# Attention, two feed-forward stages on one core: order of the outputs, of the first step, and products of zeros at the start

## The chip, the cores and the metric

The kernel runs on 1 core of one Trainium2 chip. The metric is the device time of one execution, in microseconds (us), as the median over several runs. A profile is one execution taken by the hardware profiler; its own time and its span (first to last instruction) are given beside it.

## The reference

Inputs are q, k, v of 8 batches x 8 heads x 576 positions x 64, and the weights of two feed-forward stages. What is computed, cut to its core:

```python
gamma = 1.0 - 2.0 ** (-5.0 - np.arange(H))
Dmat = np.where(rel >= 0, gamma ** rel, 0.0)           # rel = query position - key position
attn = ((q @ k.T) / sqrt(64) * Dmat) @ v               # per batch and head, no softmax
x = attn.transpose(0, 2, 1, 3).reshape(4608, 512)
h = max(max(x @ w1, x @ w2), x @ w3);  x = h @ w_out   # 512 -> 768 -> 512
a = x @ u1;  b = x @ u2;  out = ((a * b) @ u3) @ uo    # 512 -> 1024 -> 1024 -> 512
```

All arrays are fp32.

## The kernel before

The first part, up to about 184 us, is the attention. Heads are taken in pairs (32 pairs n, 64 + 64 rows of a 128-partition tile), two pairs a step, 17 steps m. Positions are cut into 4 chunks of 128 and a tail of 64. Inside a chunk the scores are computed and decayed directly; across chunks a 64x64 state per head and chunk is carried. For a pair:

- `scores(n)` (TensorE, L929, L934): products of k and q of each chunk into PSUM.
- `decay_scores(n)`, `decay_tail(n)` (VectorE, L770, L778): scores times a table of decays, into `probs`.
- `decay_values(n)` (ScalarE, L633): v times a table, into `vdec`, in two instructions a pair.
- `sum_state(n)` (TensorE, L949): products of k and `vdec` per chunk, into PSUM bank 6 (`S_STATE`).
- `make_state(n)` (VectorE, L791, L794): the running state of each chunk from these sums, 8 instructions.
- `decay_queries(n)` (GpSimd, L551): q times a table.
- `query_state(n)` (TensorE, L965): decayed queries times the state, 128x128 by 128 columns, into the output's PSUM bank.
- `values(n)` (TensorE, L976): `probs` times v, added there.
- `read_values(n)` (ScalarE, L642): the output of the pair from PSUM into `xst`, one of two buffers; it waits for the stores of pair n - 2.
- `store_x(n)` (SP, L381): two transfers of each pair's output to DRAM.

Step m takes scores, decay and state sums of pairs 2m and 2m + 1 (`made_in`), and queries, values and outputs of pairs 2m - 2 and 2m - 1 (`read_in`). From step 3 on TensorE also computes the product of u3 and uo (`wc_quarter`, L991 to L995, into bank 7, `S_WC`), so that the last two products of the reference become one. All orders are written out by hand, engine by engine, and semaphores join them; an engine takes its instructions in order. On TensorE a step is scores of both pairs, parts of the weight product, queries, state sums, values. `scores(n)` waits from pair 2 on for decays of the step before, and from pair 4 on for `x_out`, the output copies of pair n - 4. On ScalarE a step is splits of weights, `decay_values` of the next step's pairs, `read_values` of this step's.

All transfers are issued by SP, in one queue. Ahead of the steps SP issues q and k, tables, v and the k of the first pairs; in step m it issues loads of weights, k of pairs 2m + 2 and 2m + 3 (each waits for a state sum that frees its buffer), q and k of pairs 2m + 4 and 2m + 5, and then v, store, v, store: v of pairs 2m + 4 and 2m + 5, outputs of 2m - 2 and 2m - 1.

The second part, stages B, C, I and O, multiplies the tokens by the weights, each product as three products of split operands (L1026 to L1028). The change doesn't touch it.

Of the kernel before, what the change touches and what calls it, by code (L numbers as in the profile page):

```python
# [4 lines left out]
P = 128  # L5
BATCH, HEADS, SEQ, DH = 8, 8, 576, 64
# [8 lines left out]
CH = 128  # L15
NC = SEQ // CH
# [149 lines left out]
def made_in(m):  # L166
    return [n for n in (2 * m, 2 * m + 1) if n < NP]


def read_in(m):  # L170
    return [n for n in (2 * m - 2, 2 * m - 1) if n >= 0]


def quarters(m):
    if m >= STEPS - 2:
        return range(QUARTERS - 4 * (STEPS - m), QUARTERS - 4 * (STEPS - m) + 4)
    return range(2 * (m - WC_FROM), 2 * (m - WC_FROM) + 2) if m >= WC_FROM else ()
# [18 lines left out]
def build(nc, qk, vv, kk, wB, wC, wI, u3T, uo, decay, qdecay, vdecay, outT):  # L196
    f32, f32r = mybir.dt.float32, mybir.dt.float32r
# [10 lines left out]
    with ctx:  # L208
# [40 lines left out]
        o = H_AT + 4 * N * 4  # L249
# [5 lines left out]
        o = 50176  # L255
# [25 lines left out]
        o += 2 * NC * CH * 4  # L281
        state = [at(f"state{i}", [P, NC, P], f32, o + i * NC * P * 4) for i in range(2)]
        o += 2 * NC * P * 4
        assert o <= 150528

        ps = ctx.enter_context(nc.psum_tensor("ps", [P, 8, 512], f32))
# [2 lines left out]
        S_STATE, S_WC = 6, 7  # L289

        def sem(name):
            return ctx.enter_context(nc.semaphore(name))

        zeroed = sem("zeroed")
        qk_loaded = [sem(f"qk_loaded{i}") for i in range(4)]
        v_loaded = [sem(f"v_loaded{i}") for i in range(6)]
# [326 lines left out]
        def _(act):  # L623
# [14 lines left out]
            def read_values(n):  # L638
                act.wait_ge(valued, n + 1)
                if n >= 2:  # L640
                    act.wait_ge(x_stored[n % 2], 32 * (n // 2))
                nc.scalar.copy(xst[:, n % 2, :],  # L642
                               ps[:, 2 * (n % 2):2 * (n % 2) + 2, :].rearrange("p a b -> p (a b)")[:, 0:SEQ]
                               ).then_inc(x_out, 1)
# [11 lines left out]
            def read_wc(kb):  # L656
                act.wait_ge(wc_done, kb + 1)
                if kb:
                    act.wait_ge(wc_stored, 32 * kb)
                nc.scalar.copy(wcst[:, :, :].rearrange("p n c -> p (n c)"), ps[:, S_WC, :]).then_inc(wc_out, 1)  # L660
# [9 lines left out]
            def split_tokens(tau, pos):  # L670
# [11 lines left out]
                    act.wait_ge(prod, DONE[(last_of(tau - 1), USED_BY[pos])])  # L682
                nc.scalar.copy(chi[st][pos][:, :, :], raw_block(tau, pos)[:, :, :]).then_inc(c_hi, 1)  # L683

            for n in made_in(0):
                decay_values(n)
            for m in range(STEPS):
                if m in U3_SPLIT:
                    split_u3(U3_SPLIT[m])
                for i in UO_SPLIT.get(m, ()):  # L690
                    split_uo(i)
                if m in WC_READ:
                    read_wc(WC_READ[m])
                for n in made_in(m + 1):
                    decay_values(n)
                for n in read_in(m):
                    read_values(n)
                if m in P1_W_HI:
                    split_weight(P1_W_HI[m], 0)
                    split_weight(P1_W_HI[m], 1)  # L700
                if m in P1_HI:
                    split_tokens(0, P1_HI[m])
# [55 lines left out]
        def _(dve):  # L758
# [3 lines left out]
            def decay_scores(n):  # L762
                p = n % PAIRS
                dve.wait_ge(scored, n + 1)
                if n < 3:
                    dve.wait_ge(dec_loaded[n], 16)
                if n >= 4:
                    dve.wait_ge(valued, n - 3)
                for h in range(2):
                    nc.vector.tensor_tensor(  # L770
                        probs[n % 4][:, h, 0:NC * CH].rearrange("p (n c) -> p n c", c=CH),
                        ps[:, 2 * (n % 2) + h, :].rearrange("p (n c) -> p n c", c=CH),
                        dec[:, 2 * p + h, :].unsqueeze(1).broadcast_to([P, NC, CH]), ALU.mult).then_inc(decayed, 1)
# [8 lines left out]

            def make_state(n):
                p = n % PAIRS
                dve.wait_ge(state_summed, n + 2 - n % 2)
                for c in range(NC):
                    for h in range(2):
                        own = slice(h * DH, h * DH + DH)
                        new = ps[own, S_STATE, (n % 2 * NC + c) * DH:(n % 2 * NC + c + 1) * DH]
                        if c == 0:  # L790
                            nc.vector.tensor_copy(state[n % 2][own, c, own], new).then_inc(state_made, 1)  # L791
                        else:
                            dve.wait_ge(state_made, 2 * NC * n + 2 * (c - 1) + h + 1)
                            nc.vector.scalar_tensor_tensor(  # L794
                                state[n % 2][own, c, own], state[n % 2][own, c - 1, own], CHUNK_DECAY[2 * p + h], new,
                                ALU.mult, ALU.add).then_inc(state_made, 1)
# [17 lines left out]
            def split_tokens(tau, pos):  # L814
                st = tau // TILES
                dve.wait_ge(c_hi, 7 * tau + pos + 1)
                low(clo[st][pos][:, :, :], raw_block(tau, pos)[:, :, :], chi[st][pos][:, :, :]).then_inc(c_lo, 1)

            for i in range(4):
                nc.vector.memset(probs[i][0:TAIL, :, NC * CH:SEQ], 0.0).then_inc(zeroed, 1)  # L820
            for i in range(2):
# [2 lines left out]
            for m in range(STEPS):  # L824
                for n in made_in(m):
                    decay_scores(n)
                for n in made_in(m):
                    decay_tail(n)
                if m in U3_SPLIT:
                    split_u3(U3_SPLIT[m])  # L830
                for i in UO_SPLIT.get(m, ()):
                    split_uo(i)
                if m in P1_W_LO:
                    split_weight(*P1_W_LO[m])
                if m in P1_LO:
                    split_tokens(0, P1_LO[m])
                for n in made_in(m):
                    make_state(n)

            merge = {B: ALU.max, I: ALU.mult}  # L840

# [76 lines left out]
        def _(pe):  # L918
            def scores(n):
                pe.wait_ge(qk_loaded[n % 4], 16 * (n // 4 + 1))  # L920
                if n >= 2:
                    pe.wait_ge(decayed, 3 * (n - n % 2))
                if n >= 4:
                    pe.wait_ge(x_out, n - 3)
                for c in range(NC):
                    for h in range(2):
                        own = slice(h * DH, h * DH + DH)
                        keys = SEQ + c * CH
                        nc.tensor.matmul(ps[:, 2 * (n % 2) + h, c * CH:(c + 1) * CH], qks[n % 4][own, keys:keys + CH],  # L929
                                         qks[n % 4][own, c * CH:(c + 1) * CH],  # L930
                                         start=(c == 0), stop=(c == NC - 1), skip_group_check=True)
                for h in range(2):
                    own = slice(h * DH, h * DH + DH)
                    last = nc.tensor.matmul(ps[:, S_TAIL[h], (n % 2) * TAIL:(n % 2 + 1) * TAIL],  # L934
                                            qks[n % 4][own, KQ_COLS - CH:KQ_COLS], qks[n % 4][own, SEQ - TAIL:SEQ],
                                            start=True, stop=True, skip_group_check=True)
                last.then_inc(scored, 1)

            def sum_state(n):
                pe.wait_ge(v_decayed, 2 * n + 2)  # L940
                pe.wait_ge(k_loaded[n % 2], 16 * (n // 2 + 1))
                if n >= 2:
                    pe.wait_ge(state_made, 2 * NC * (n - n % 2))
                for c in range(NC):
                    for h in range(2):
                        own = slice(h * DH, h * DH + DH)
                        keys = c * P + h * DH
                        at_ = (n % 2 * NC + c) * DH
                        last = nc.tensor.matmul(ps[own, S_STATE, at_:at_ + DH],  # L949
                                                ks[n % 2][:, keys:keys + DH], vdec[n % 2][:, c, own],  # L950
                                                start=(c == 0), stop=(c == NC - 1), skip_group_check=True)
                last.then_inc(state_summed, 1)
# [28 lines left out]
            def wc_quarter(i):  # L981
# [15 lines left out]
                if part == 3:  # L997
                    last.then_inc(wc_done, 1)

            pe.wait_ge(zeroed, 6)  # L1000
            for m in range(STEPS):
                for n in made_in(m):
                    scores(n)
                for i in quarters(m):
                    wc_quarter(i)
                for n in read_in(m):
                    query_state(n)
                for n in made_in(m):
                    sum_state(n)
                for n in read_in(m):  # L1010
                    values(n)
# [102 lines left out]
```

## Time and profile before

| | |
|---|---|
| median of 3 runs | 1265.27 us (1263.46 to 1265.35) |
| profiled execution, its own time | 1261.15 us |
| its span | 1259.4 us |
| granted TensorE clock, mean | 0.997 |
| PE busy | 1223.0 us (97%), 8288 matmuls |
| DVE busy | 787.4 us (63%) |
| ACT busy | 486.6 us (39%) |
| POOL busy | 407.2 us (32%) |

PE is TensorE, DVE is VectorE, ACT is ScalarE, POOL is GpSimd, SP is SyncE, whose queue of transfers is SPq. Busy times are shares of the whole span; the attention part and the four stages after it have limits of their own, so the rows below are taken from the attention part. "DMA share" is the mean busy share of 16 DMA engines and can read a little over 1.

### The profile page before, as it was taken

What the parts mean: (1) busy time and instruction counts of PE and PEld (TensorE: products, weight loads), DVE (VectorE), ACT (ScalarE), POOL (GpSimd) and SP (SyncE); (2) the same over time, 40 slices, a digit from 0 to 9 for tenths busy, and PEclk for the clock granted to TensorE, in tenths of its full rate; (3) what the DMA queues carried; (4) which work ended last, traced back from release to release, by engine and by line L of the source; (5) the groups of instructions that cost most, each with busy time, mean ns of one, the idle gap of its engine ahead of it and who ended that gap; (6) DMA issues with size and microseconds to landing.
All of it is one profiled execution on the core that took longest, in us unless ns stands there. A gap on an engine that the chain in (4) does not pass through costs nothing. (4 is left out here: it accounts for less than half of the span.)

```text
span 1259.4 us, 21123 instructions
## 1 busy us (share of the span) xinstructions
PE 1223.0 (97%) x8288; PEld 1205.0 (96%) x8288; DVE 787.4 (63%) x1198; ACT 486.6 (39%) x771; POOL 407.2 (32%) x216
## 2 busy tenths in 40 slices
PE   6999999999999999999999999999999999899999
PEld 6898889999999999998999999999999999899998
DVE  6877748764646363659698777453535366766563
ACT  3343434422323232325554534242423234455441
POOL 2334218320202020063778571202020117266540
PEclk9999999999999999999999999999999999899999
DMA  9999945020202021053555441313132142344441
GB/s 365 347 350 345 336 144 192 26 101 26 100 26 94 32 82 45 27 175 119 178 197 178 156 154 51 107 51 101 60 103 95 70 174 94 145 156 156 152 157 63
DMA packets 87827, 174.15 MB, mean 138 GB/s; under 512 B 9648, under 2 KB 58416, under 8 KB 87728
## 3 DMA queue, kind: packets, MB, share of 16 engines
q1 hardware_dynamic: 87728, 172.80, 38.7%
q8 instruction: 66, 1.08, 0.3%
q14 instruction: 33, 0.27, 0.1%
HBM read 109.32 MB, written 63.44 MB: 137 GB/s over the span
## 5 line engine op out<-in xcount | busy, mean ns | idle before, releaser
L1026 PE MATMUL ps<-chi,whi 128*128 128x384 f32 x2016 | 676.4, 336 | 15.9 <-DVE wlo L760 8.3
L1028 PE MATMUL ps<-chi,wlo 128*128 128x384 f32 x2016 | 674.7, 335 | 0.0
L1027 PE MATMUL ps<-clo,whi 128*128 128x384 f32 x2016 | 674.6, 335 | 0.0
L551 POOL TENSOR_TENSOR raw<-raw,raw 128x768 f32<-128x768 f32 (+2 forms) x96 | 265.5, 2784 | 592.1 <-DMA raw<-xd 209.7
L1026 PEld LDWEIGHTS ps<-chi,whi 128*128 128x128 f32 x2016 | 379.3, 188 | 21.1 <-issue 10.6
L1027 PEld LDWEIGHTS ps<-clo,whi 128*128 128x128 f32 x2016 | 379.3, 188 | 0.0
L1028 PEld LDWEIGHTS ps<-chi,wlo 128*128 128x128 f32 x2016 | 379.3, 188 | 0.0
L760 DVE TENSOR_TENSOR clo<-raw,chi 128x768 fp32r<-128x768 f32 (+2 forms) x168 | 239.5, 1453 | 24.0 <-ACT chi L683 23.9
L683 ACT CAST chi<-raw 128x768 fp32r<-128x768 f32 (+2 forms) x168 | 180.3, 1081 | 84.7 <-PE ps L1028 59.2
L753 ACT COPY w<-ps 128x384 f32<-128x384 f32 x126 | 60.5, 480 | 229.4 <-PE ps L1028 227.9
L736 ACT COPY u<-ps 128x384 f32<-128x384 f32 x126 | 60.7, 481 | 176.3 <-PE ps L1028 174.9
L884 DVE TENSOR_TENSOR h<-ps,u 128x384 f32<-128x384 f32 x66 | 36.7, 555 | 126.6 <-PE ps L1028 126.6
L857 DVE TENSOR_TENSOR h<-ps,w 128x384 f32<-128x384 f32 x66 | 36.6, 554 | 108.9 <-PE ps L1028 103.7
L857 DVE TENSOR_TENSOR w<-ps,w 128x384 f32<-128x384 f32 x60 | 33.4, 557 | 87.6 <-PE ps L1028 86.6
L717 ACT COPY s<-ps 128x384 f32<-128x384 f32 x126 | 60.6, 481 | 66.8 <-PE ps L1028 65.7
L760 DVE TENSOR_TENSOR wlo<-wraw,whi 128x768 fp32r<-128x768 f32 (+4 forms) x42 | 81.8, 1947 | 1.6 <-POOL wraw L551 1.2
L551 POOL TENSOR_TENSOR qdec<-qks,qtab 128x512 f32<-128x512 f32 x32 | 44.5, 1412 | 112.5 <-PE ps L965 100.0
L728 ACT COPY h<-ps 128x384 f32<-128x384 f32 x66 | 31.6, 479 | 93.5 <-PE ps L1028 88.2
L884 DVE TENSOR_TENSOR u<-ps,u 128x384 f32<-128x384 f32 x60 | 33.2, 554 | 52.5 <-PE ps L1028 52.5
L551 POOL TENSOR_TENSOR wraw<-w,wraw 128x256 f32<-128x256 f32 (+2 forms) x21 | 24.0, 1144 | 112.3 <-DMA w<-wC 79.3
L633 ACT ACTIVATE vdec<-vs,vtab 128x256 f32<-128x256 f32 x64 | 28.2, 500 | 72.2 <-PE ps L949 37.1
L929 PE MATMUL ps<-qks 64*128 64x128 f32 x512 | 38.6, 292 | 14.2 <-ACT xst L642 7.3
(41 smaller groups left out, 847.0 us busy)
## 6 DMA issues: line engine op xcount, KB each, us to landing
qks<-qk SPq DMA_DIRECT2D x32, 576.0 KB, 6.8
gd<-h SPq DMA_DIRECT2D x96, 192.0 KB, 1.9
raw<-gd SPq DMA_DIRECT2D x24, 768.0 KB, 6.0
hd<-h SPq DMA_DIRECT2D x72, 192.0 KB, 1.9
raw<-hd SPq DMA_DIRECT2D x24, 576.0 KB, 5.7
vs<-vv SPq DMA_DIRECT2D x32, 320.0 KB, 7.2
raw<-xd SPq DMA_DIRECT2D x24, 384.0 KB, 5.6
x2d<-h SPq DMA_DIRECT2D x48, 192.0 KB, 2.3
```

The lines of the kernel that those rows point to most:

```text
L551: return nc.gpsimd.tensor_tensor(out_, a, b, op)
L683: nc.scalar.copy(chi[st][pos][:, :, :], raw_block(tau, pos)[:, :, :]).then_inc(c_hi, 1)
L717: nc.scalar.copy(sbuf_s[it % 2][:, :], ps[:, X[it % 2], 0:N]).then_inc(s_made, 1)
L736: nc.scalar.copy(sbuf_u[it % 2][:, :], ps[:, X[it % 2], 0:N]).then_inc(u_made, 1)
L753: nc.scalar.copy(sbuf_w[it % 2][:, :], ps[:, X[it % 2], 0:N]).then_inc(w_made, 1)
L760: return nc.vector.tensor_tensor(out_, whole, hi.bitcast(f32), ALU.subtract)
L857: nc.vector.tensor_tensor(to[:, :], ps[:, Z[g % 2], 0:N], sbuf_w[g % 2][:, :], ALU.add).then_inc(sum22, 1)
L884: nc.vector.tensor_tensor(to[:, :], ps[:, Z[g % 2], 0:N], sbuf_u[g % 2][:, :], ALU.add).then_inc(sum12, 1)
L929: nc.tensor.matmul(ps[:, 2 * (n % 2) + h, c * CH:(c + 1) * CH], qks[n % 4][own, keys:keys + CH], qks[n % 4][own, c * CH:(c + 1) * CH], sta ...
L1026: nc.tensor.matmul(to, w1, x1, start=(start and k == 0), stop=False, skip_group_check=True)
L1027: nc.tensor.matmul(to, w1, x2, start=False, stop=False, skip_group_check=True)
L1028: last = nc.tensor.matmul(to, w2, x1, start=False, stop=(k == KH[st] - 1), skip_group_check=True)
```

## The change

Four edits. (a) On ScalarE, in every step, `read_values` of this step stands ahead of `decay_values` of the next. (b) In step 0, TensorE takes scores and state sums pair by pair, scores(0), sum_state(0), scores(1), sum_state(1), and VectorE makes state 0 between the decay of scores 0 and that of scores 1; the state sums of pair 1 go into bank `S_WC`, and each state of step 0 waits only for its own sum. (c) A small tile `warm` is cleared by VectorE first; TensorE multiplies its zeros 7 times ahead of everything (128x128 by 128 columns, fp32, into `S_WC`) and 4 times after sum_state(0). (d) ScalarE copies one column of `warm` as its first instruction.

```diff
@@ tiles and semaphores
+        warm = at("warm", [P, CH + 2], f32, o); o += (CH + 2) * 4
+        warmed = sem("warmed")
@@ scalar
+            act.wait_ge(warmed, 1)
+            nc.scalar.copy(warm[:, CH + 1:CH + 2], warm[:, CH:CH + 1])
             for n in made_in(0):
                 decay_values(n)
             for m in range(STEPS):
...
                 if m in WC_READ:
                     read_wc(WC_READ[m])
+                for n in read_in(m):
+                    read_values(n)
                 for n in made_in(m + 1):
                     decay_values(n)
-                for n in read_in(m):
-                    read_values(n)
@@ vector, make_state(n)
-                dve.wait_ge(state_summed, n + 2 - n % 2)
+                bank = S_WC if n == 1 else S_STATE
+                dve.wait_ge(state_summed, n + 2 - n % 2 if n >= 2 else n + 1)
...
-                        new = ps[own, S_STATE, (n % 2 * NC + c) * DH:(n % 2 * NC + c + 1) * DH]
+                        new = ps[own, bank, (n % 2 * NC + c) * DH:(n % 2 * NC + c + 1) * DH]
@@ vector
+            nc.vector.memset(warm[:, :], 0.0).then_inc(warmed, 1)
...
                 for n in made_in(m):
                     decay_scores(n)
+                    if n == 0:
+                        make_state(n)
...
                 for n in made_in(m):
-                    make_state(n)
+                    if n:
+                        make_state(n)
@@ tensor, sum_state(n)
+                bank = S_WC if n == 1 else S_STATE
...
-                        last = nc.tensor.matmul(ps[own, S_STATE, at_:at_ + DH],
+                        last = nc.tensor.matmul(ps[own, bank, at_:at_ + DH],
@@ tensor
+            def run_idle(count):
+                for _ in range(count):
+                    nc.tensor.matmul(ps[:, S_WC, 0:CH], warm[:, 0:CH], warm[:, 0:CH], start=True, stop=True,
+                                     skip_group_check=True)
+
+            pe.wait_ge(warmed, 1)
+            run_idle(7)
             pe.wait_ge(zeroed, 6)
             for m in range(STEPS):
                 for n in made_in(m):
                     scores(n)
+                    if m == 0:
+                        sum_state(n)
+                        run_idle(4 * (n == 0))
...
-                for n in made_in(m):
+                for n in made_in(m) if m else ():
                     sum_state(n)
```

## Rows read from the trace of the kernel before

**Rows 1.** Waits of PE, 0 to 200 us: waiter, releaser, us, times, longest.
```profile
PE ps L929 <- ACT xst L642: 7.3, 7, 2.6
...
PE ps L965 <- DVE probs L770: 3.0, 2, 2.7
```

**Rows 2.** Busy us by stretch; last three columns: granted clock, DMA share, GB/s.
```profile
0.00:46.12 46.12, 32.48 (x468) 30.50 (x469) 33.54 (x86) 17.76 (x31) 12.52 (x12) 1.00 0.96 365
5.00:43.00 38.00, 28.86 (x398) 26.96 (x394) 28.99 (x76) 15.52 (x26) 9.20 (x7) 1.00 1.04 401
46.00:74.00 28.00, 27.55 (x352) 25.36 (x348) 21.39 (x66) 9.54 (x17) 9.95 (x10) 1.00 1.01 359
74.00:84.00 10.00, 9.91 (x139) 9.19 (x139) 6.50 (x22) 2.92 (x6) 3.57 (x5) 1.00 0.89 286
84.00:116.00 32.00, 30.03 (x418) 27.78 (x417) 24.57 (x71) 15.14 (x26) 12.84 (x10) 1.00 1.04 387
```

**Rows 3.** Timeline of PE: start, us, instruction group, idle before it and its releaser.
```profile
8.87 2.08 PE L929 MATMUL ps<-qks 64*128 64x128 f32 x16 [2.01 <-DMA qks<-qk]
25.09 1.16 PE L929 MATMUL ps<-qks 64*128 64x128 f32 x16 [1.09 <-ACT xst L642]
31.07 2.15 PE L976 MATMUL ps<-probs,vs 128*64 128x128 f32 x40
35.87 1.16 PE L929 MATMUL ps<-qks 64*128 64x128 f32 x16 [2.64 <-ACT xst L642]
...
109.84 1.16 PE L929 MATMUL ps<-qks 64*128 64x128 f32 x16 [1.67 <-ACT xst L642]
...
152.09 1.16 PE L929 MATMUL ps<-qks 64*128 64x128 f32 x16 [0.48 <-ACT xst L642]
```

**Rows 4.** Timeline of ACT around steps 3, 9 and 10.
```profile
32.82 0.91 ACT L633 ACTIVATE vdec<-vs,vtab 128x256 f32<-128x256 f32 x2 [4.41 <-DMA vs<-vv]
34.29 0.91 ACT L633 ACTIVATE vdec<-vs,vtab 128x256 f32<-128x256 f32 x2 [0.57 <-DMA vs<-vv]
35.11 1.15 ACT L642 COPY xst<-ps 128x576 f32<-128x576 f32 x2
...
98.02 0.64 ACT L642 COPY xst<-ps 128x576 f32<-128x576 f32 x1 [0.20 <-DMA xd<-xst]
108.27 0.91 ACT L633 ACTIVATE vdec<-vs,vtab 128x256 f32<-128x256 f32 x2 [0.59 <-DMA vs<-vv]
```

**Rows 5.** Timeline: state sums of step 0, decays of step 1, queries of step 3.
```profile
11.19 1.97 PE L949 MATMUL ps<-vdec,ks 128*64 128x64 f32 x32
17.23 2.48 DVE L770 TENSOR_TENSOR probs<-ps,dec 128x512 f32<-128x512 f32 x4
41.12 1.90 PE L965 MATMUL ps<-qdec,state 128*128 128x128 f32 x16
```

**Rows 6.** Timeline of SP's queue: k of pairs 4, 5; outputs of pairs 0, 1, 17.
```profile
21.59 0.81 SPq L369 DMA_DIRECT2D ks<-kk  x2
24.97 0.81 SPq L381 DMA_DIRECT2D xd<-xst  x2
26.29 0.91 SPq L381 DMA_DIRECT2D xd<-xst  x2
100.01 1.09 SPq L381 DMA_DIRECT2D xd<-xst  x2
```

**Rows 7.** Issue to landing (us, last) of these: 21.59; 24.97 (two); 26.29, second; 100.01, second.
```profile
ks<-kk SPq DMA_DIRECT2D x1, 256.0 KB, 6.4
xd<-xst SPq DMA_DIRECT2D x1, 192.0 KB, 6.2
xd<-xst SPq DMA_DIRECT2D x1, 96.0 KB, 8.2
...
xd<-xst SPq DMA_DIRECT2D x1, 96.0 KB, 8.3
...
xd<-xst SPq DMA_DIRECT2D x1, 192.0 KB, 8.4
```

## The prediction

> **What bounds the kernel now.** I read the waits of TensorE first, then a table by stretch, then the rows around each wait, last the landing times of the transfers. The change touches only the attention part, the first 184 us, so the first question is what that part has to give. TensorE waits there 7 times, 7.3 us in all, for the copy of the outputs on ScalarE (L642), and twice, 3.0 us, for decayed scores on VectorE [rows 1]; two waits for the first q and k remain, which nothing here moves. By stretch [rows 2]: up to 46.12 us, the first product of step 4, TensorE is busy 32.48 us, so 13.6 us are open. The same rows show the second limit. The DMA share is 1.04 from 5 to 43 us, at 401 GB/s, and 1.04 again from 84 to 116; it is 1.01 from 46 to 74 and 0.89 from 74 to 84. I take 1.04 as full: there transfers land at a pace that no engine can hasten, and that decides most of what follows.
>
> Each step (two pairs) is scores, parts of the weight product (from step 3), queries, state sums, values. The 7 waits are 1.09, 2.64, 0.37, 0.26, 1.67, 0.83 and 0.48 us, all at the first scores of a step; the first two, the 1.67 and the last are shown [rows 3]. Why ScalarE is late there is in its rows [rows 4]: it takes the decayed values of the next step first, which wait for v to land (32.82, 34.29 and 108.27 us); the copies of the outputs come right behind (35.11), although the values were done at 31.07 + 2.15 = 33.2.
>
> **The change part by part.**
>
> (1) *Outputs ahead of decayed values.* Nothing is added or removed: two groups on ScalarE change places in 14 steps. A copy waits for its values and, from pair 2 on, for the stores of the pair two before it, which free its buffer. Behind it wait the decayed values of the next step, and for them TensorE's state sums of that step. That cover is long: first scores at 35.87, sums not before 41.12 + 1.90 = 43.0 [rows 3, 5], 7 us against the 1.15 us of two copies and 1.8 us of four decays [rows 4]. So I cost the delay at nothing; without the cover it would be 1.15 us a step. What is won is the wait, as far as nothing else is late, and what can be late are the stores.
>
> Step 3 (the 2.64 us): the store of pair 0 is two transfers, issued from 24.97 to 25.8; the second, of 96 KB, starts about 25.4 and lands 8.2 us later, at 33.6; that of pair 1 (26.29 on) at 26.75 + 8.3 = 35.05 [rows 6, 7]. After the change they are issued earlier, but behind the same transfers in a queue that is full from 5 to 43 us, so I leave both landings where they are. Then the copy of pair 2 runs from 33.6 to 34.2, that of pair 3 from 35.05 to 35.65, and the scores of pair 7 start at 35.75 instead of 35.87 + 1.13 = 37.0: **-1.25 us**. The other end: if those stores landed 3 us earlier, as their copies are made (part 2), VectorE is next, and the gain is 2.9.
>
> On this the Trainium skill ("DMA: Bandwidth & Descriptors", Queues, rings and completion order) says that each DMA engine takes its descriptors in the order of its ring. The trace bears it out only in part: the 192 KB transfer of pair 0's store took 6.2 us from 24.97, to 31.2, and so landed ahead of the v at 32.82, which stands before it in the program; the 96 KB one did not [rows 4, 7]. By the rule the term is -1.25; without it, up to -2.9.
>
> Later steps: 0.37, 0.26, 0.83 and 0.48 us go, since SP issues v, store, v, store, and there the copies waited on the second v and its decay. At 109.84 the second transfer of pair 17's store (100.01 on) lands at 100.6 + 8.4 = 109.0 [rows 6, 7]: scores of pair 21 at 109.0 + 0.6 + 0.05 = 109.65 instead of 109.84 + 1.14 = 110.98, which is 1.33 of the 1.67. Sum: 0.37 + 0.26 + 1.33 + 0.83 + 0.48 = **-3.27 us**. This supposes that landings move forward with TensorE. There is room for it before 84 us: (1.04 - 1.01) x 28 + (1.04 - 0.89) x 10 = 2.3 us of DMA time [rows 2] against a lead of 1.25 + 0.37 + 0.26 = 1.9. Bounds: nothing beyond 0.37 where the queue holds, all 3.61 where it doesn't.
>
> (2) *First step pair by pair.* On TensorE the state sums of pair 0 move ahead of the scores of pair 1; on VectorE the state of pair 0 moves ahead of the decay of pair 1's scores; pair 1's sums get a PSUM bank that the weight product doesn't use before step 3. In the kernel before, VectorE made both states after both sums, which held the decay of pair 2's scores until 17.23 [rows 5]. With state 0 out of the way, inside an idle stretch of VectorE, that decay can start at about 15, queries 1.3 us later and step 2 at about 21.9 instead of 25.09, copies included. The earlier sum also frees the k buffer sooner: SP can issue k of pair 2 ahead of the rest, and its place in the full queue is unchanged. In step 2 VectorE's states (4 us after sums that end at 19.6) let the decays of pair 4 start at 23.6; before, they followed the scores, 25.09 + 1.35 = 26.4: this is the 2.9 of the other end above. Then loads set the pace: k of pair 4 (21.59 on) lands at 21.59 + 6.4 = 28.0 [rows 6, 7]; 1.2 us of sums and 2.2 of values behind it end at 31.4 instead of 33.2. There TensorE meets the store of pair 0, at 33.6, so this part is covered whole by step 3's wait: **0**. The new wait in order, sums of pair 0 for v and k, holds the scores of pair 1 up to 0.5 us longer than 8.87 [rows 3], inside the 2.2 us between 31.4 and 33.6. Bounds +0.5 and the -2.9 above.
>
> (3) *Eleven products of zeros, a clear, a table load.* No row has these products; the nearest is L965, 128x128 by 128, 16 in 1.90 us or 0.12 each [rows 5]. Scores took 2.08 us for 16 at the start and 1.16 later [rows 3], 1.8 times, so 0.21 each. Seven take 1.5 us, while TensorE waits for the first q; four take 0.5 to 0.9 ahead of scores 1. If they raise the pace early, scores 1 save 2.08 - 1.16 = 0.9 and state sums 1.97 - 1.15 = 0.8; if not, they cost 0.9. The granted clock reads 1.00 (2.4 GHz) in all these stretches, and durations alone show the slow start. Either way it ends ahead of the same 2.2 us: **0**. The waits of ScalarE, TensorE and VectorE on the clear come in stretches where all three wait for the first loads.
>
> Sum: -1.25 - 3.27 = -4.5 us. The profiled execution took 1261.15 (span 1259.4 and 1.75 around it), so one like it would take 1256.6. The median shown is 1265.27, 4.1 above it, and I take the difference over: **1260.8 us**. Bounds: +0.5 - 1.25 - 0.37 = -1.1 and -2.9 - 3.6 = -6.5, that is 1264.2 and 1258.8.
>
> **The rivals.**
>
> A. *The transfers take it back.* Landings from 84 to 116 us don't move: scores of pair 21 come at 109.65 whatever was won before, so 1.33, and about half of 0.83 + 0.48 after it. Total -2.0: 1263.3. For it: share 1.04 there. Against: the 2.3 us of room ahead.
>
> B. *The stores of pairs 0 and 1 land early.* -6.5: 1258.8. For it: the 192 KB transfer that overtook. Against: the 96 KB one.
>
> C. *The store's round trip becomes the loop.* With copies first, copy, issue, landing and next copy close a loop. Pair 17's took from 98.02, where ScalarE did wait for a store, to 109.0, 11.0 us [rows 4, 6, 7]. If earlier requests only lengthen the queue and every step costs that, the 11 steps from 46.12 to 162.3 take 121 instead of 116.2 us: +4.8 - 1.25 = +3.5: 1268.8, slower. It decides from 10.7 us a step. Against: pair 0's loop is 9.3 by the same count, and 98.02 is the only such wait in this part.
>
> D. *TensorE slows after its longer idle.* It would idle from 31.4 to 34.3, 2.9 us; after 2.64 us the scores still took 1.16 for 16 [rows 3]. Running as at the start would cost scores and sums 0.9 + 0.8 = 1.7 us: total -2.8: 1262.5. The Trainium skill ("TensorE: Matmul & The Clock Gate", Part 1) has idle stretches put the clock back to 1.2 GHz; no row here shows it fall, and none has so long an idle behind work.
>
> **How the numbers follow.** Forecast (-3 to -6) 0.52, A 0.20, B 0.13, C 0.07, D 0.08. What a measurement of this kernel tells from no change is about 0.2%, 2.5 us. The forecast and B lie beyond it but for a spread of 1.5 us, A within, D on the line: faster 0.67, same 0.26, slower 0.07. The forecast's own range is 1259.3 to 1262.3; the range reaches to B and over A and D, 1258.4 to 1264.6, and leaves C out.
>
> **What would show it.** Right: TensorE's waits for L642 shrink from 7.3 to some 3.5 us, most of it one wait that ends at 34.3; the copies there wait for stores; step 2 begins at 21.9, step 4 at 44.8. Wrong: scores of pair 20 not before 108 (A), step 4 before 43.6 (B), copies waiting for stores in most steps (C), 16 scores in 2 us after 34 (D).

## The result, and the profile after

The change is faster. Over 8 runs each the median went from 1264.03 us (1262.15 to 1267.47) to 1257.26 us (1253.05 to 1261.24), ratio 0.9948, 95% interval 0.9926 to 0.9970. The medians lie 6.8 us apart where 4.5 were forecast; 1257.3 lies 1.1 us under the range, whose lower end is 1258.4. The profiled execution took 1258.55 us, its span is 1256.8, its mean granted clock 0.995.

The waits of PE from 0 to 200 us after the change (waiter, releaser, us in total, times, longest), against [rows 1]:

```profile
PE ps L938 <- ACT xst L644: 2.8, 6, 1.4
PE ps L975 <- DVE probs L774: 2.4, 2, 1.3
PE ps L959 <- ACT vdec L635: 1.9, 1, 1.9
PE ps L938 <- DVE probs L782: 1.4, 1, 1.4
```

The wait for the outputs fell from 7.3 to 2.8 us. The start has new ones: state sums for decayed v, scores of pair 2 for decays. PE's timeline at the first scores of steps 2, 3, 10, 11 and 12, against [rows 3]:

```profile
23.43 1.16 PE L938 MATMUL ps<-qks 64*128 64x128 f32 x16
33.77 1.16 PE L938 MATMUL ps<-qks 64*128 64x128 f32 x16 [1.42 <-ACT xst L644]
35.32 1.75 PE L938 MATMUL ps<-qks 64*128 64x128 f32 x16 [0.21 <-ACT xst L644]
108.14 1.16 PE L938 MATMUL ps<-qks 64*128 64x128 f32 x16 [0.39 <-ACT xst L644]
109.64 1.16 PE L938 MATMUL ps<-qks 64*128 64x128 f32 x16 [0.17 <-ACT xst L644]
118.67 1.16 PE L938 MATMUL ps<-qks 64*128 64x128 f32 x16
128.79 1.16 PE L938 MATMUL ps<-qks 64*128 64x128 f32 x16
```

Scores of pair 21 stand at 109.64 (before, 110.98). And a step without any wait now lasts 128.79 - 118.67 = 10.12 us; before, such a step lasted 87.50 - 77.25 = 10.25 us:

```profile
77.25 1.16 PE L929 MATMUL ps<-qks 64*128 64x128 f32 x16
87.50 1.16 PE L929 MATMUL ps<-qks 64*128 64x128 f32 x16
```

ACT at step 3 and step 4, against [rows 4], and under it the same step 4 before:

```profile
32.99 0.64 ACT L644 COPY xst<-ps 128x576 f32<-128x576 f32 x1 [4.37 <-DMA xd<-xst]
34.53 0.64 ACT L644 COPY xst<-ps 128x576 f32<-128x576 f32 x1 [0.91 <-DMA xd<-xst]
...
45.03 0.64 ACT L644 COPY xst<-ps 128x576 f32<-128x576 f32 x1 [6.38 <-PE ps L986]
```

```profile
43.74 1.71 ACT L633 ACTIVATE vdec<-vs,vtab 128x256 f32<-128x256 f32 x4 [5.11 <-PE ps L949]
45.36 0.62 ACT L642 COPY xst<-ps 128x576 f32<-128x576 f32 x1
```

At 32.99 the copy of pair 2 waits for the store of pair 0, as forecast. In step 4 before, where no wait is listed, the copy still came behind 1.7 us of decays and ended at 45.98, just when the values ended.

### The profile page after: what moved, and what is told of

The parts are those of the page before. It is cut to its first block and busy times, and to the rows that moved or that the text cites. A ratio compares the mean times of both kernels' runs of the same rounds, so it can differ in the third digit from the quotient of the medians.

```text
span 1256.8 us, 21169 instructions
## 1 busy us (share of the span) xinstructions
PE 1228.0 (98%) x8310; PEld 1209.3 (96%) x8310; DVE 792.6 (63%) x1199; ACT 485.7 (39%) x772; POOL 406.9 (32%) x216
## 5 line engine op out<-in xcount | busy, mean ns | idle before, releaser
L553 POOL TENSOR_TENSOR raw<-raw,raw 128x768 f32<-128x768 f32 (+2 forms) x96 | 264.0, 2770 | 591.9 <-DMA raw<-xd 208.1
L764 DVE TENSOR_TENSOR clo<-raw,chi 128x768 fp32r<-128x768 f32 (+2 forms) x168 | 246.6, 1495 | 32.2 <-ACT chi L685 32.1
L764 DVE TENSOR_TENSOR wlo<-wraw,whi 128x768 fp32r<-128x768 f32 (+4 forms) x42 | 83.0, 1975 | 1.6 <-POOL wraw L553 1.2
L553 POOL TENSOR_TENSOR qdec<-qks,qtab 128x512 f32<-128x512 f32 x32 | 45.2, 1434 | 108.3 <-PE ps L975 95.8
L553 POOL TENSOR_TENSOR wraw<-w,wraw 128x256 f32<-128x256 f32 (+2 forms) x21 | 24.2, 1151 | 113.6 <-DMA w<-wC 79.5
L644 ACT COPY xst<-ps 128x576 f32<-128x576 f32 x32 | 20.5, 639 | 83.5 <-PE ps L986 65.2
L553 POOL TENSOR_TENSOR wraw<-wraw 128x256 f32<-128x256 f32 (+2 forms) x42 | 51.8, 1234 | 1.6
```

Of the source, the lines that this page charges most:

```text
L553: return nc.gpsimd.tensor_tensor(out_, a, b, op)
L764: return nc.vector.tensor_tensor(out_, whole, hi.bitcast(f32), ALU.subtract)
```

## The experiments

Sixteen runs were made, each beside the kernel before on the same chip; e13 to e16 are single executions, the others medians of 6 to 12. Each ratio is to the kernel before in the same set, with its 95% interval. Stage B's first product marks the end of the attention part; step 5's first scores mark the end of the start. In their profiles (us):

| kernel | step 5 | stage B | from there to the end | span |
|---|---|---|---|---|
| before; e13; e14 | 56.37; 57.81; 57.87 | 184.74; 188.83; 187.09 | 1074.7; 1074.1; 1076.2 | 1259.4; 1262.9; 1263.3 |
| change; e1; e15; e16 | 56.04; 57.70; 56.90; 55.74 | 181.55; 183.55; 181.59; 180.98 | 1075.3; 1074.6; 1073.0; 1071.9 | 1256.8; 1258.1; 1254.6; 1252.9 |
| e2; e3; e4 | 57.26; 56.89; 56.04 | 181.15; 184.04; 180.97 | 1073.4; 1069.9; 1067.9 | 1254.5; 1253.9; 1248.9 |
| e5; e6; e7; e8 | 57.76; 57.28; 56.35; 57.07 | 186.71; 182.64; 181.81; 182.62 | 1068.8; 1070.9; 1070.2; 1069.7 | 1255.5; 1253.5; 1252.0; 1252.3 |
| e9; e10; e11; e12 | 58.10; 57.68; 57.06; 56.76 | 183.68; 182.52; 184.87; 181.72 | 1069.4; 1070.3; 1070.7; 1070.1 | 1253.1; 1252.8; 1255.6; 1251.8 |

**The change taken apart.** e1 is the change as it is.

> The whole change again. In the profile read so far the granted clock fell to 0.50 around 36 to 39 us, just behind the wait for the store of pair 0, and step 4 began at 45.9 instead of the 44.8 forecast. Theory 1 (order: the gain is the order on ScalarE, the start is covered by that store): 4 to 5 us faster, all runs alike. Theory 2 (start: step 0 pair by pair and the zeros are worth some us of their own): 6 to 9 us faster. Theory 3 (clock: executions differ by whether TensorE falls to half pace in the first 43 us): two groups, those with a mean clock of 0.997 near 1254, those with 0.993 to 0.995 near 1260.

Measured: 1257.84 us, ratio 0.9951 (0.9934 to 0.9967), 5.5 us against the 1263.31 of before in this set, between theories 1 and 2. There are no two clean groups: a mean clock of 0.996 goes with 1254.0 as with 1259.9. So theory 3 doesn't explain the spread here, though in the first eight runs the four at 0.996 to 0.997 took 1253.1 to 1256.0 and the four at 0.993 to 0.995 1258.6 to 1261.2.

e2, the order alone:

```diff
+                for n in read_in(m):
+                    read_values(n)
                 for n in made_in(m + 1):
                     decay_values(n)
-                for n in read_in(m):
-                    read_values(n)
```

> Only the outputs ahead of the decayed values on ScalarE, nothing of the first step, no zeros. Theory 1: the same gain as the whole change, 4 to 5 us, step 4 at about 44.9. Theory 2: 3 to 4 us less gain than the whole change. Theory 3: no fall of the clock at the start, since the waits keep the places they had; spread of runs as before.

Measured: 1258.90 us, 0.9958 (0.9942 to 0.9974), 4.4 us under before. Theory 1 holds for the size; step 4 began at 45.99, not 44.9. Theory 3 fails, since in e2's profile the granted clock is 0.50 from 18.3 to 21.8 us. Between 56 and 180 us TensorE is busy throughout, where the kernel before leaves 3.9 us open (columns as in [rows 2]; e2, then before):

```profile
56.00:180.00 124.00, 123.99 (x1639) 114.56 (x1636) 89.70 (x271) 49.02 (x89) 44.08 (x35) 1.00 0.87 311
```

```profile
56.00:180.00 124.00, 120.11 (x1582) 110.42 (x1578) 88.72 (x266) 46.79 (x84) 41.19 (x35) 1.00 0.87 309
```

e3 is the change with the old order on ScalarE (the diff of e2 taken back):

> The whole change but for the order on ScalarE, which is the old one (decayed values first). Theory 1: no gain, within 1 us of before. Theory 2: 2 to 4 us faster. Theory 3: as theory 1, with single executions slower by 2 to 5 us where the clock falls.

Measured: 1260.45 us, 0.9982 (0.9971 to 0.9993): 2.9 us, as theory 2 has it, though the interval (0.9 to 3.7 us) nearly reaches theory 1. e4 leaves out `run_idle(7)` and `run_idle(4 * (n == 0))`:

> The whole change without the eleven products of zeros. Theory 1: the same as the whole change. Theory 2: up to 2 us less gain, if the zeros are what counts at the start. Theory 3: fewer executions with a fall of the clock (the clock is raised later, so there is less to lose in the idle stretches before 12 us), median 1 to 3 us below the whole change.

Measured: 1256.94 us, 0.9934 (0.9914 to 0.9954), 0.9 us under e1 with overlapping intervals. The zeros win nothing that shows. The mean clocks of e4's runs are 0.996 to 0.999, those of e1's 0.993 to 0.996, which agrees with theory 3's fewer falls of the clock; the gain in time that it expects is not shown.

**A turn in stage O.** In e3 and e4 the part from stage B on was 5 to 7 us shorter than in the change and e1. The rows around 1085 us show the largest piece of it: GpSimd subtracts one block of tokens from another (L551, L553) while VectorE makes the lower half of the last weight, its split (L760, L764). Which of the two comes first is the turn. Before, the change, and e4 (start, duration, group):

```profile
1086.85 4.13 POOL L551 TENSOR_TENSOR raw<-raw,raw 128x1536 f32<-128x1536 f32 x1 [15.37 <-DMA raw<-gd]
1087.57 5.57 DVE L760 TENSOR_TENSOR wlo<-wraw,whi 128x2048 fp32r<-128x2048 f32 x1
...
1093.28 0.66 PE L1026 MATMUL ps<-chi,whi 128*128 128x384 f32 x1 [3.38 <-DVE wlo L760]
```

```profile
1084.52 4.01 POOL L553 TENSOR_TENSOR raw<-raw,raw 128x1536 f32<-128x1536 f32 x1 [15.48 <-DMA raw<-gd]
1085.11 5.57 DVE L764 TENSOR_TENSOR wlo<-wraw,whi 128x2048 fp32r<-128x2048 f32 x1
```

```profile
1082.31 2.29 DVE L764 TENSOR_TENSOR wlo<-wraw,whi 128x2048 fp32r<-128x2048 f32 x1
1082.39 5.56 POOL L553 TENSOR_TENSOR raw<-raw,raw 128x1536 f32<-128x1536 f32 x1 [16.09 <-DVE clo L764]
```

Whichever of the two starts second takes 5.6 us; where a wait keeps them apart (e6), they take 2.29 and 3.51:

```profile
1085.05 2.29 DVE L766 TENSOR_TENSOR wlo<-wraw,whi 128x2048 fp32r<-128x2048 f32 x1
1087.57 3.51 POOL L553 TENSOR_TENSOR raw<-raw,raw 128x1536 f32<-128x1536 f32 x1 [18.59 <-DVE wlo L766]
```

If the split is second, TensorE waits 3.4 us for it, and its granted clock falls to 0.50 (1.2 GHz), from 1092.4 to 1099.3 before and from 1090.4 to 1093.8 in the change. The Trainium skill ("SBUF — State Buffer", SBUF: two separate sides) says that these two engines share a port pair: of a VectorE instruction with two inputs from SBUF and a GpSimd one that reads SBUF, whichever starts first holds it for the whole instruction. These rows agree: before, the subtraction ends at 1086.85 + 4.13 = 1090.98 and the split 2.2 us later. One wait makes the turn sure, in e5 to e12:

```diff
 def combine(tau, i):                     # GpSimd
...
     if i == 0:
         for k in (0, 1):
             pool.wait_ge(raw_loaded[k], 16 * (tau + 1))
+        if tau == O * TILES + 1:
+            pool.wait_ge(w_lo, 2 * NW)
...
```

e5, the kernel before with it, and e6, the change with it:

> The kernel before with one wait more: GpSimd starts the first subtraction of the second tile of stage O only when VectorE has split the last weight. In the profiles read so far these two meet at about 1085 us: where GpSimd starts first (before, the change, e1, e2) VectorE's split takes 5.6 us, TensorE waits 3.4 us and its clock falls for 3.4; where VectorE starts first (e3, e4) it takes 2.3 and there is no wait. Theory 1 (turn: a part of what the medians moved beyond the waits of the attention part is this chance): 4 to 5 us faster than before, if it always loses the turn, and a smaller spread. Rival (the change itself moved it): as much faster as the change with the same wait is faster than the change.

> The whole change with the same wait. Theory 1: 2 to 3 us faster than the change as it is, which wins the turn in some executions only, so that against e5 about 3 to 3.5 us are left, what the trace shows at the first product of stage B. Rival: 4 to 5 us faster than the change, 6 us against e5.

Measured: e5 1259.73 us (1256.79 to 1262.50), 0.9972 (0.9955 to 0.9989); e6 1254.37 (1253.89 to 1255.62), 0.9938 (0.9916 to 0.9960). So the wait wins 3.6 us before and, against other sets, 2.9 to 3.5 in the change. Against e5, e6 is 5.4 us faster, not 3 to 3.5: theory 1 is wrong about what moved the medians, and the rival is nearer, though its 4 to 5 and 6 are not reached. e13 to e16 test the same from the other side, four more profiles of the two unchanged kernels:

> The kernel before, unchanged, one more profile. Theory (chance adds to the change: the end of the attention part moves by 3 to 4 us, and the turn in stage O falls to GpSimd nearly always before and in some executions after): stage B begins at 184.5 to 187, and GpSimd's subtraction comes ahead of VectorE's split at about 1087. Rival (no such difference): the turn is lost as often as after the change.

> As e13: a second profile of the kernel before, unchanged, with the same expectations of both theories.

> The whole change, unchanged, one more profile. Theory: stage B begins at 181 to 183.5, the turn in stage O is won in some of these looks (then the part after the first product of stage B takes about 1070 us, else 1074 to 1075). Rival: lost here as in the kernel before, and the rest takes 1074 to 1075 in both.

> As e15: a second profile of the whole change, unchanged, with the same expectations of both theories.

Measured: 1264.64, 1265.07, 1256.39 and 1254.71 us. GpSimd starts first in all four, as in the other three profiles of these kernels, so in these seven executions the turn explains nothing of the difference. What does is the attention part itself: stage B began at 184.74, 188.83 and 187.09 before, and at 181.55, 183.55, 181.59 and 180.98 after. The profile that the prediction was made from had the shortest waits of the three. From 56 to 180 us, the waits for outputs in it, in e13 and in e14, then in the change's first profile and in e16:

```profile
PE ps L929 <- ACT xst L642: 3.6, 5, 1.7
```

```profile
PE ps L929 <- ACT xst L642: 4.9, 5, 2.0
```

```profile
PE ps L929 <- ACT xst L642: 4.4, 3, 2.1
```

```profile
PE ps L938 <- ACT xst L644: 1.2, 4, 0.4
```

```profile
PE ps L938 <- ACT xst L644: 0.8, 3, 0.5
```

**What holds the start back.** e7 is e4 with the wait, e8 the change with the wait and two buffers more:

```diff
+        xst0 = at("xst0", [P, 2, SEQ], f32, comb_base[B])
...
-                if n >= 2:
+                if n >= 4:
                     act.wait_ge(x_stored[n % 2], 32 * (n // 2))
-                nc.scalar.copy(xst[:, n % 2, :],
+                nc.scalar.copy((xst if n >= 2 else xst0)[:, n % 2, :],
```

(the stores of pairs 0 and 1 read `xst0` too).

> The change without its eleven products of zeros, with the same wait. Theory (zeros only move falls of the clock about): 0.5 to 2 us faster than e6, with no fall of the clock in the first 45 us. Rival (the zeros help): 1 us slower than e6.

> The whole change with the same wait, and two output buffers more for pairs 0 and 1, so that the copies of pairs 2 and 3 wait for no store. The prediction had step 3 wait for that store and cost it 1.25 us. Theory as the traces now suggest (VectorE's splits of steps 2 to 4 decide when step 5 begins, about 56): step 3 begins 1 to 1.5 us earlier, at about 32.4, step 5 and the end don't move (within 0.5 us of e6). Rival (the store decides): step 5 and the end 1.2 us earlier.

Measured: e7 1254.64 us, 0.9941 (0.9918 to 0.9965), as e6; its profile has no fall of the clock before 699 us, as expected, and no gain in time from that. e8 1254.11, 0.9935 (0.9915 to 0.9955), as e6. In e8 the copy of pair 2 waits for its values, not for a store:

```profile
32.51 0.64 ACT L647 COPY xst<-ps 128x576 f32<-128x576 f32 x1 [2.62 <-PE ps L989]
```

Step 3 begins at 33.39 (e6: 33.75), step 5 at 57.07 (57.28). So the store decided at most 0.4 us, less than profiles of one kernel differ there (33.66 to 34.31 in the four of the change): the values themselves come just ahead of it. The end doesn't move, as the theory has it. In e1, e15 and e6 the queries of steps 3 and 4 wait 0.6 to 1.2 us each for VectorE, which had worked through the splits of the last weight; in e16 those of step 4 wait 0.9, in the change's first profile none. e9 gives those four splits to GpSimd:

```diff
 for m in range(STEPS - 1):               # GpSimd
...
+    for i in UO_SPLIT.get(m, ()):
+        pool.wait_ge(uo_hi, i + 1)
+        add(uolo[:, 2 * i:2 * i + 2, :], uoraw[:, 2 * i:2 * i + 2, :],
+            uohi[:, 2 * i:2 * i + 2, :].bitcast(f32), ALU.subtract).then_inc(uo_lo, 1)
     for n in made_in(m):
         decay_queries(n)
@@ VectorE
-                for i in UO_SPLIT.get(m, ()):
-                    split_uo(i)
```

> The whole change with the wait of e6, and the four lower halves of the last weight (steps 2 and 3) made by GpSimd instead of VectorE. Theory (VectorE's chain through these splits sets when step 5 begins, and so took what the start won): the queries of step 4 wait no more for decayed scores, step 5 begins at 54 to 55.5 instead of 57.3, the end 1.5 to 2.5 us before e6. Rival (transfers set it): step 5 and the end where e6 has them, within 0.5 us, and TensorE waits for q or the copies there instead.

Measured: 1253.23 us (1251.66 to 1254.92), 0.9916 (0.9898 to 0.9934), 1.1 us under e6, but from another set. VectorE now idles ahead of the decays of step 4, and they follow the scores:

```profile
44.54 0.48 DVE L802 COPY state<-ps 64x64 f32<-64x64 f32 x2 [3.41 <-PE ps L958]
...
48.90 1.29 DVE L780 TENSOR_TENSOR probs<-ps,dec 128x512 f32<-128x512 f32 x2 [0.37 <-PE ps L942]
```

Step 4 lasts 58.10 - 47.53 = 10.6 us instead of 57.28 - 46.01 = 11.3 in e6, so VectorE did hold it. But step 4 itself came 1.5 us late, behind waits for q (1.5 us in 3 up to 60 us) and outputs (2.5 in 4), and step 5 not at 54 to 55.5. Two things in e9 make it late. Its clock was at 0.50 from 17.9 to 24.7 us, twice as long as in e6 (19.0 to 22.4). And the edit itself holds the transfers: GpSimd takes two splits (5.66 us) ahead of the decayed queries that free the buffers of q, and SP waits for those before it loads the next q. The stores of pairs 2 and 3 stand behind that load; the first of them was issued 4.0 us after its copy had ended at 35.70, where e6 has 0.4 us. GpSimd's splits and that store in the timeline, and SP's wait from 20 to 50 us:

```profile
30.62 5.66 POOL L553 TENSOR_TENSOR uolo<-uoraw,uohi 128x1024 fp32r<-128x1024 f32 x2 [7.13 <-ACT uohi L656]
...
39.66 0.90 SPq L383 DMA_DIRECT2D xd<-xst  x2
```

```profile
SPq L360 <- POOL qdec L553: 6.8, 4, 4.3
```

So TensorE waits for q and copies, as the rival has it, but not for the transfers that the kernel had before the edit. What would hold the start with VectorE free and GpSimd not loaded stays open.

e10 (order alone, with the wait) and e11 (start alone, with the wait):

> Only the order on ScalarE, with the wait of e6. Theory (the order is nearly the whole gain, 3.6 us of waits and 0.12 us a step that no list of waits shows): 4 to 5 us faster than e5, within 1 us of e6. Rival (the first step and the zeros carry a good part): 2 us or more slower than e6.

> The first step pair by pair and the zeros, the old order on ScalarE, with the wait of e6. Theory: within 1.2 us of e5. Rival: 2 us or more faster than e5.

Measured: e10 1254.31 us, 0.9923 (0.9904 to 0.9941), equal to e6. e11 1257.32, 0.9951 (0.9933 to 0.9970), 2.4 us under e5, from another set with wide overlap. The order alone gives the whole gain, as far as these sets can tell; what the start gives by itself, 2.9 and 2.4 us in two sets, doesn't add to it. e12 joins e4, e8 and e9, with the wait:

> What the runs point to, together: the change without the zeros, with the wait of e6, the buffers of e8 and the splits of e9 on GpSimd. If the splits are what holds the start back: 2 to 4 us faster than e6, 8 to 10 us faster than the kernel before. If transfers hold it: as e7, about 1254.5.

Measured: 1253.20 us (1251.34 to 1260.61), 0.9920 (0.9893 to 0.9947), the same as e9 and 1.2 us under e6, short of the 2 to 4 expected if the splits are what holds the start. Its stores of pairs 2 and 3 come late as in e9 (from 38.55 on). Versions with the new order and the wait (e6 to e10, e12) are all some 2.5 to 4.5 us under the change; among them nothing can be told apart.

## Why the prediction was right and wrong

*The step that failed: the size of the later steps, and the level.* Right is the mechanism: decays of v ahead of the copies cost TensorE its waits, and the order removes them. Mis-sized is the term: -3.27 us were forecast; from step 5 to stage B the three profiles before take 129.5 us on average (128.4, 131.0, 129.2), the four after 125.3 (125.5, 125.9, 124.7, 125.2): **-4.2 us**. Up to step 10, 2.0 us of this are won (53.9 to 51.9 us on average), where 0.37 + 0.26 + 1.33 were forecast; behind it 2.2 (75.6 to 73.4), where 0.83 + 0.48 were.

Three things were missing from the term. First, I summed the waits that the timeline lists. A step without a listed wait still went from 10.25 us to 10.12: the copy behind the decays ended as the values ended, and the next scores could not overlap them. The order does this, for e2 and e10 have the short step too, and e3 and e11, with the old order, don't. Ten steps make 1.2 us. Second, the waits were those of one execution, 3.6 us behind 56; in two others they are 4.4 and 4.9, and in e13 the clock fell to 0.50 in this part too (112.9 to 116.3). Against these, more waiting stayed than the 0.34 us forecast: listed are 1.2, 1.2, 0.5 and 0.8 in the four profiles after.

*Pair 21 at 109.65.* It came at 109.64, behind the store that was forecast, but the agreement is luck. The sum supposes a lead of 1.9 us ahead of it, with which it should have come at about 107.8; step 8 began at 87.43 against 87.50, a lead of 0.1, and the store landed at 108.78 instead of 109.03. So the sign of rival A was there, scores of pair 20 not before 108: they came at 108.14, and in e1, e15 and e16 at 110.16, 108.16 and 107.58. A's total of -2.0 us is refuted by the medians all the same, since the steps behind gave more than either had. (The store issued at 100.01 is that of pair 15, not 17, in the rows and in the prediction; it is the one that the copy of pair 17 waits for, so the argument stands. And of the lead, 0.26 us is at 97.97, behind the 84 us up to which room was counted.)

*Step 3 and the store, -1.25 us.* The wait stands where it was forecast, for the stores forecast: 32.99 and 34.53 against 33.6 and 35.05. The second transfer of pair 0's store was issued 1.5 us earlier and landed 0.6 us earlier; in the seven profiles of the two kernels it was issued between 23.3 and 25.8 and landed between 32.8 and 33.5, so its landing hardly follows its issue, and rival B is out. What failed here is what I let come after it: I took TensorE to be the bound from step 4 on, and costed VectorE's chain at 2.9 us earlier. It came 0.9 earlier (decays of pair 4 at 25.59 in place of 26.46, where 23.6 was forecast, and of step 3 at 37.99 in place of 38.86), and step 5 began at 56.6 on average of four instead of 57.35 of three: **-0.8 us**. That is less than profiles of one kernel differ there (55.74 to 57.70 after). The sum in part (2) was wrong in its first term: decays of pair 2 can't start at 15, since the third part of their table lands at 16.64 (VectorE at 16.73 waits for it, against 17.23 before, [rows 5]). So step 2 began at 23.43 instead of 21.9, and the values of step 2 ended at 32.35 instead of 31.4, with 0.6 us left to the store in place of 2.2.

```profile
16.73 2.48 DVE L774 TENSOR_TENSOR probs<-ps,dec 128x512 f32<-128x512 f32 x4 [0.42 <-DMA dec<-decay]
```

*The first step and the zeros at 0.* Right beside the order (e2 and e10 equal e1 and e6 within their intervals, and so do e4 and e7), but not by the cover that I named alone, as e8 shows: without that store nothing more is won. With the old order the start gives 2.4 to 2.9 us.

*Rival D, the clock.* It came, at a chance of 0.08, in one of four profiles. In the change's first profile the granted clock stands at 0.50 of full, its 1.2 GHz level, from 35.7 to 39.1 us, behind the idle stretch at 33 us, and the second scores took 1.75 us for 16 (columns as in [rows 2]):

```profile
35.00:36.00 1.00, 0.79 (x11) 0.71 (x11) 0.88 (x5) 1.00 (x4) 0.00 (x0) 0.86 1.00 388
36.00:37.00 1.00, 1.00 (x15) 1.00 (x12) 0.88 (x5) 1.00 (x3) 0.00 (x0) 0.50 1.05 421
38.00:39.00 1.00, 1.00 (x4) 0.81 (x3) 1.00 (x2) 0.66 (x1) 0.00 (x0) 0.50 0.98 397
```

The idle stretch was 1.4 us; 2.6 us in the kernel before and 1.8 in e16 brought no fall there, so the length of one stretch, by which I priced D, doesn't decide. The rule of the Trainium skill ("TensorE: Matmul & The Clock Gate", Part 1) that idle stretches bring 1.2 GHz back agrees with these rows. e1, e15 and e16 have no fall at that place. e1 and e15 have one near 20 us, and so have e13 and e14, profiles of the kernel before (e15, then e13):

```profile
19.40:22.60 3.20, 3.20 (x42) 3.08 (x43) 0.08 (x1) 0.00 (x0) 2.09 (x2) 0.50 1.02 400
20.80:24.00 3.20, 3.20 (x46) 3.08 (x46) 0.64 (x3) 1.49 (x4) 1.79 (x2) 0.50 1.02 412
```

Up to stage B the clock is at 0.50 for 6.8, 3.4, 3.4 and 0 us in the four profiles after and for 0, 6.8 and 3.4 in the three before, the same on average: falls cost both kernels, and D takes nothing from the change that shows. Nor was a fall unseen in the profile that I read: one begins at 1092.4, in TensorE's wait of 3.38 us in stage O.

*The rest of the kernel, taken as constant.* It was not: 1075.0 us on average of three before, 1073.7 of four after. This term was put at nothing, and the 1.3 us is left open. The clock is at 0.50 for 6.8, 6.8 and 10.2 us there before and for 6.8 in each profile after, which makes some 0.6 us (an estimate: half of the difference of the averages); no run ties it to the change, and with the turn made sure the rest is no longer before (1068.8 in e5) than with the change (1069.4 to 1070.9 in e6 to e10). Together -0.8 - 4.2 - 1.3 = -6.3 us, between the 6.8 and 5.5 us of the medians in the two sets.

*The level.* I put the difference on the median of the three runs shown, 1265.27. The eight runs of the comparison have 1264.03, later sets of 17, 24 and 11 have 1263.31, 1263.34 and 1263.79. The level was 1.2 us too high, and this alone is more than the 1.1 us by which the result left the range: from 1264.03 the range is 1257.2 to 1263.4, and 1257.26 lies just inside. The forecast from it, 1259.5, would still have been 2.3 us off, for the terms above.

## What to carry to other kernels

On an engine that takes its work in order, what frees another engine's buffer goes ahead of preparation for the next step. Here it paid in every step, also in those where no wait is listed, since work that ends just in time keeps the next from overlapping; and e9, which put two splits ahead of what frees the buffers of q, held two stores back by some 4 us. A gain at a start that is fed by transfers can end at the next load; follow it through every engine and every table up to the point where the pipeline is full before counting it. One profile gives the places of the waits well and their sizes badly: size them, and the level, from several executions.

## What the runs showed that was not expected

An instruction of VectorE on 128x2048 took 2.29 us or 5.57, by whether GpSimd had started a subtraction up to 0.7 us earlier; with the wait of TensorE behind it one GpSimd wait wins 3.6 us of 1263, more than half of what the whole change does, and it can be had in the kernel before too (e5). Behind the seven products of zeros the first 16 scores took 1.44 us in the change's profile and 2.08 in e1, with a granted clock recorded as 1.00 in both up to 8 us; nothing in the time follows from it.
